# Attention, cosine mixing and gated attention on one core: the order of the steps for all engines, written out

## The chip, the cores and the metric

One core of one Trainium2 chip runs the whole program. The metric is the device time of one execution in microseconds (us), as the median of several runs. Durations and waits are read from one profiled execution of the kernel.

## The reference

The program computes three layers in a row, all in fp32, for 4 batches of 576 tokens with 512 channels:

```
# layer 1: 8 heads of 64; heads 0-3 see the last 32 tokens, heads 4-7 every 32nd token
scores = where(mask[h], q @ k.T / 8, -1e9);  x = softmax(scores) @ v
# layer 2: mixing with a cosine and a sine
theta = x @ w_theta;  zr, zi = x * cos(theta), x * sin(theta)
u = x + w_tok_r @ zr + w_tok_i @ zi
x = u + max(u @ w_ch, 0)
# layer 3: 4 causal attention heads ("experts"), two of which are chosen for each token
w = softmax over the 2 largest of (x @ w_gate)
out = sum over e of w[e] * softmax(causal(x @ wq[e] @ (x @ wk[e]).T / 8)) @ (x @ wv[e]) @ wo[e]
```

## The kernel before, in words

**Tiling.** Tokens lie in five tiles (four of 128 and one of 64), channels in four chunks of 128. Large products are split: each fp32 operand is kept as a high and a low part, and `split_matmuls` (L1271 and on; the matmul itself is L1278) issues three matmuls, hi by hi, hi by lo and lo by hi, in place of one. Transposes and the attention products are plain fp32 matmuls.

**Software pipeline.** Layer 1 of batch r runs together with layer 3 of batch r-1. The program is a PROLOGUE (layers 1 and 2a of batch 0, and the loading and splitting of the weights), three times a BODY (the channel product, q, k, v and layer 3 of one batch, with layers 1 and 2a of the next), and an EPILOGUE (the rest for the last batch). Each is one list of steps. Every engine walks the same list through its own `emit` and does its share of each step, in the order of the list; a step that has nothing for an engine is passed over. So the list fixes the order of the instructions on each of the queues (PE, DVE, ACT, POOL, and SP for the loads), and nothing reorders them. Data goes from engine to engine by semaphores.

**PSUM.** There are three pairs of buffers, `wide` (2 banks each), `turned` and `acc`. `Counts.take` hands them out by turns in the order of the list, and a step on PE waits until the use before of its buffer has been read.

**The steps.** A unit of attention is ("s1", pair) in layer 1, with four units, or ("s3", group, pair) in layer 3, with five: group 0 holds token tiles 0 to 2, group 1 tile 3, group 2 tile 4 with both pairs of heads at once. The steps of a unit:

- prep, tail: PE transposes q and k (L1311, L1322). copied: ACT and DVE copy them out (L878, L1028).
- scores: masks and products on PE (L1335, L1350; in layer 3 L1371, L1376).
- max: DVE, for one of two heads (L1045, L1049). exp: ACT, with the sums (L895, L902).
- norm: DVE makes the reciprocal of the sum. For head 0 it also scales the probabilities itself (L1070, L1080); for head 1 POOL scales them (L814, L823).
- turn: PE transposes the probabilities (L1391, L1404), ACT and DVE copy them out to `pt` (L910, L1093).
- values: PE multiplies them by v (L1421, L1447), DVE copies the result out (L1106, or L1116 and L1118). xu (layer 1): ACT and POOL split it into high and low parts (L921, L833).

The other steps are large products on PE with an eviction of their own: channel, qk, v, theta, out and wtok. Their eviction stands in the list as a step of its own, `("done", ...)`. theta's eviction is three DVE operations (L1125, L1128, L1130), of which the second frees the buffer. A theta product has four chunks, each of three matmuls, and can be cut: ("theta", m, 0, 2) is the first two chunks. trig is ACT (L942, L943), products is a transpose on PE (L1489) and two DVE products (L1140, L1142), split is ACT and POOL (L958, L840), wave and mix are the token products on PE. piece splits a part of the weights (ACT L999, then DVE L1254, or POOL L828 for theta's); SP loads piece n+3 once piece n is split. warm is a number of matmuls whose result nobody reads. rank, gexp and gate choose the experts (DVE, ACT, DVE).

**What sets the order.** `attention_steps` (L89) writes the body by slots: in slot i unit i is ahead (scores, max, exp, norm) and unit i-1 behind (turn, values), and four gaps of the slot are filled from FILL (L262) with the large products. `slot_of_s3` (L137) is the slot of layer 3; `alone_steps` (L178) does the same for the prologue. A gap's product is followed at once by its eviction (`at_once`, L85), except in `slot_of_s3`, which puts the evictions of its first three gaps at the slot's end:

```
    steps = [("turn",) + behind + (0,), ("scores",) + ahead, ("max",) + ahead + (0,), ("max",) + ahead + (1,),
             ("exp",) + ahead + (0,)]
    steps += gap[0] + [("turn",) + behind + (1,), ("norm",) + ahead + (0,), ("exp",) + ahead + (1,)]
    steps += gap[1] + [("values",) + behind] + gap[2] + [("norm",) + ahead + (1,)]
    return steps + done(gap[0] + gap[1] + gap[2]) + at_once(gap[3])
```

The EPILOGUE is already a list that is written out, in both kernels the same.

## Time and profile before

| | us |
|---|---|
| median of 3 runs (lowest to highest) | 575.8 (575.56 to 576.6) |
| the profiled execution | 575.45 |
| its span, first to last instruction | 573.7 |
| PE busy | 545.1 (95%) |
| PE's weight loads (PEld) busy | 467.0 (81%) |
| DVE busy | 348.9 (61%) |
| ACT busy | 259.6 (45%) |
| POOL busy | 130.4 (23%) |

The page cuts the span into 40 slices; the granted clock of TensorE reads 9, which is 90% or more, in all of them, and its mean is 0.999. The profiled execution lies 1.75 us above its span, and 0.35 us below the median of the runs. A PE that shows as busy isn't one at its peak: matmuls overlap, and the ends that the profile shows are modelled. The prologue runs to about 98 us, each body takes 134.8 us, and the epilogue starts at about 502 us.

### The profile page before, as it was taken

The page shows a single profiled execution, that of the slowest core. Times are in us where ns is not written, and L with a number is a line of the kernel's source. Part 1 is how long each engine was busy: PE and PEld are TensorE (multiplying, and loading weights), DVE is VectorE, ACT ScalarE, POOL GpSimd, SP SyncE. Part 2 cuts the span into 40 slices and gives each one's busy share as a digit, 9 for nine tenths or more (in the row PEclk, how much of TensorE's full clock was granted, in tenths as well). Part 3 has the DMA queues.
Part 4 walks back from the last instruction along what each step waited for, and adds up shares of the span by engine and source line. Part 5 has one row for each costly group of instructions (what it writes and reads, how often), then busy time and mean ns, then how long its engine had stood idle before and what let it go on. Part 6 is the DMA issues. An engine that isn't in the chain of part 4 may idle for free.

```text
span 573.7 us, 11679 instructions
## 1 busy us (share of the span) xinstructions
PE 545.1 (95%) x4473; PEld 467.0 (81%) x4473; DVE 348.9 (61%) x843; ACT 259.6 (45%) x775; POOL 130.4 (23%) x131
## 2 busy tenths in 40 slices
PE   6999999999999999999999999999999999999986
PEld 5777889989866799899876689999976679998764
DVE  1677856675888622476678741567677952343683
ACT  2874734555533541355553542255643454121453
POOL 4550710022221250011321152011131126000110
PEclk9999999999999999999999999999999999999999
DMA  9742046221000114211000012331000010000002
GB/s 224 178 115 77 1 112 158 67 49 27 2 0 1 38 47 112 66 43 30 14 1 2 19 65 55 83 83 23 22 1 1 1 75 10 1 2 1 0 1 83
DMA packets 73413, 27.13 MB, mean 47 GB/s; under 512 B 68624, under 2 KB 68624, under 8 KB 73360
## 3 DMA queue, kind: packets, MB, share of 16 engines
q1 hardware_dynamic: 68848, 24.38, 16.7%
q10 hardware_dynamic: 4512, 2.02, 1.3%
q8 instruction: 36, 0.59, 0.4%
q14 instruction: 17, 0.14, 0.1%
HBM read 21.67 MB, written 4.72 MB: 46 GB/s over the span
## 4 chain that ended last, share of the span: by engine, by line
PE 74%; DVE 15%; ACT 5%; issue 3%; POOL 2%; POOLq 0%; DVEq 0%; ACTq 0%
PE acc L1278 33%; PE wide L1278 14%; PE wide L1350 4%; PE turned L1447 4%; PE turned L1391 3%; PE wide L1371 3%; PE turned L1404 2%; DVE xt L1106 2%; PE turned L1421 2%; DVE nmax L1049 2%; PE turned L1489 2%; PE turned L1311 2%; ACT probs L902 2%; PE wide L1335 1%; DVE probs L1080 1%
## 5 line engine op out<-in xcount | busy, mean ns | idle before, releaser
L814 POOL TENSOR_TENSOR probs<-probs,rec 96x768 f32<-96x768 f32 (+1 forms) x16 | 21.7, 1354 | 204.2 <-DVE rec L1064 204.2
L910 ACT ACTIVATE pt<-turned 128x384 f32<-128x384 f32 (+3 forms) x64 | 30.8, 481 | 77.4 <-PE turned L1404 41.4
L895 ACT ACTIVATE probs<-wide,nmax 96x128 f32<-96x128 f32 (+1 forms) x176 | 61.5, 369 | 9.0 <-DVE nmax L1045 8.9
L823 POOL TENSOR_TENSOR probs<-probs,weight 128x128 f32<-128x128 f32 (+4 forms) x36 | 26.9, 767 | 145.9 <-DVE weight L1087 145.9
L902 ACT ACTIVATE probs<-wide,nmax 128x128 f32<-128x128 f32 (+4 forms) x72 | 39.0, 553 | 36.2 <-DVE nmax L1049 25.6
L1278 PE MATMUL wide<-w_tok_hi,z_hi 128*128 128x288 f32 x216 | 47.4, 300 | 0.0
L1278 PE MATMUL wide<-w_tok_hi,z_lo 128*128 128x288 f32 x216 | 46.0, 293 | 0.0
L1278 PE MATMUL wide<-w_tok_lo,z_hi 128*128 128x288 f32 x216 | 45.9, 293 | 0.0
L1049 DVE TENSOR_REDUCE nmax<-wide 128x1 f32<-128x128 f32 (+4 forms) x72 | 33.1, 512 | 13.1 <-PE wide L1376 13.0
L840 POOL TENSOR_TENSOR z_lo<-absf,z_hi 128x512 fp32r<-128x512 f32 x20 | 26.3, 1317 | 63.9 <-ACT z_hi L958 63.9
L1278 PE MATMUL acc<-xu_hi,w_ch_hi 128*128 128x288 f32 x128 | 39.3, 307 | 1.0 <-DVE xu_lo L1176 0.9
L1140 DVE TENSOR_TENSOR absf<-turned,absf 128x512 f32<-128x512 f32 (+1 forms) x20 | 13.7, 686 | 42.6 <-PE turned L1489 42.6
L1278 PE MATMUL acc<-x_hi,w_qk_hi 128*128 128x288 f32 x128 | 39.6, 309 | 0.0
L1045 DVE TENSOR_REDUCE nmax<-wide 96x6 f32<-96x768 f32 (+1 forms) x32 | 27.8, 879 | 17.0 <-PE wide L1350 17.0
L1278 PE MATMUL acc<-xu_hi,w_ch_lo 128*128 128x288 f32 x128 | 37.7, 295 | 0.0
L1278 PE MATMUL acc<-x_lo,w_qk_hi 128*128 128x288 f32 x128 | 37.7, 295 | 0.0
L1278 PE MATMUL acc<-xu_lo,w_ch_hi 128*128 128x288 f32 x128 | 37.7, 294 | 0.0
L1278 PE MATMUL acc<-x_hi,w_qk_lo 128*128 128x288 f32 x128 | 37.7, 294 | 0.0
L895 ACT ACTIVATION_READ_ACCUMULATOR probs<-wide,nmax 96x1 f32 (+1 forms) x176 | 36.8, 209 | 0.0
L1093 DVE COPY pt<-turned 128x288 f32<-128x288 f32 (+4 forms) x72 | 31.9, 452 | 7.2 <-PE turned L1404 4.9
L1278 PE MATMUL acc<-w_theta_hi,xu_hi 128*128 128x512 f32 (+1 forms) x80 | 35.8, 447 | 0.2 <-DVE turns L1128 0.2
L1278 PEld LDWEIGHTS wide<-w_tok_lo,z_hi 128*128 128x128 f32 x216 | 34.4, 188 | 0.0
(190 smaller groups left out, 1458.9 us busy)
## 6 DMA issues: line engine op xcount, KB each, us to landing
raw_q<-in_q SPq DMA_DIRECT2D x32, 128.0 KB, 2.4
out<-o_sb SPq DMA_DIRECT2D x16, 256.0 KB, 2.0
raw_k<-in_k SPq DMA_DIRECT2D x28, 128.0 KB, 2.5
...
stage<-in_moe_w_theta ACTq DMA_DIRECT2D x2, 512.0 KB, 7.5
...
```

Source lines behind the costliest of these rows:

```text
L814: g.tensor_tensor(pr, pr, rec[0:rows, 1, 0:nt].unsqueeze(2).broadcast_to([rows, nt, w]), ALU.mult).then_inc(s["probs_pool"], 1)
L823: ins = g.tensor_tensor(pr, pr, weight[:, j:j + 1].broadcast_to([P, n]), ALU.mult)
L840: g.tensor_tensor(z[1][:, chunk, :], src[:, m, :], z[0][:, chunk, :].bitcast(F32), ALU.subtract).then_inc(s["zl"], 1)
L895: e = a.activation(probs[0:rows, hh, t * P:t * P + w], wide[slot][0:rows, t * P:t * P + w], ACT.Exp, bias=nmax[0:rows, hh, t:t + 1], accum ...
L902: e = a.activation(probs[:, hh, to0:to0 + n], wide[slot][:, at0:at0 + n], ACT.Exp, bias=nmax[:, hh, j:j + 1], accum_out=sums[:, hh, j:j + 1])
L910: ins = a.activation(dst, src, ACT.Copy)
L1045: v_.tensor_reduce(nmax[0:rows, hh, 0:nt], src, AX.X, ALU.max, negate=True)\
L1049: ins = v_.tensor_reduce(nmax[:, hh, j:j + 1], wide[u[0]][:, at0:at0 + TOK[m][1] + TOK[m][2]], AX.X, ALU.max, negate=True)
L1093: ins = v_.tensor_copy(dst, src)
L1278: ins = mm(place, lhs[x], rhs[y](cols), start=first and n == 0, stop=last and n == 2)
L1350: ins = mm(wide[slot][0:n, t * P:t * P + k1 - k0], qt[hd, rows * t:rows * t + n], kt[hd, k0:k1], start=False, stop=True, skip_group_check= ...
L1447: ins = mm(turned[slot][hh * HD:(hh + 1) * HD, to:to + rows], v3[0:n, j, e * HD:(e + 1) * HD], pt[0:n, hh, x:x + rows], start=j == 0, stop ...
```

## The change

The functions that put the lists together are gone, and PROLOGUE and BODY stand there step by step. Both lists hold the same steps as before, with the same arguments (131 and 210 of them); only their order is another, and with it the order of the instructions of every engine, the turns of the PSUM buffers and the point at which each wait stands. SP's order in the body stays as it was. `program`, the EPILOGUE and every instruction are untouched.

```diff
-def attention_steps(units, before, fill):
...
-def slot_of_s3(ahead, behind, gap):
...
-def alone_steps(units, early):
...
-PROLOGUE = [("warm", 3, "acc", 1)] + [PREP[0] + ("acc",)] + PREP[1:] \
...
+PROLOGUE = [
+    ("warm", 3, "acc", 1), ("prep", "s1", 0, 0, "acc"), ("copied", "s1", 0, 0), ("tail", "s1", 0, 0),
+    ("scores", "s1", 0, 0), ("max", "s1", 0, 0, 0), ("max", "s1", 0, 0, 1), ("warm", 1, "acc", 1),
+    ("prep", "s1", 1, 0, "acc"), ("exp", "s1", 0, 0, 0), ("warm", 6, "turned", 0), ("copied", "s1", 1, 0),
+    ("tail", "s1", 1, 0, 2), ("exp", "s1", 0, 0, 1), ("scores", "s1", 1, 0), ("norm", "s1", 0, 0, 0),
+    ("norm", "s1", 0, 0, 1), ("turn", "s1", 0, 0, 0), ("warm", 1, "acc", 1), ("max", "s1", 1, 0, 0), ("piece", 0),
+    ("turn", "s1", 0, 0, 1), ("max", "s1", 1, 0, 1), ("exp", "s1", 1, 0, 0), ("values", "s1", 0, 0),
+    ("prep", "s1", 2, 0, "acc"), ("norm", "s1", 1, 0, 0), ("exp", "s1", 1, 0, 1), ("copied", "s1", 2, 0),
+    ("tail", "s1", 2, 0, 2), ("turn", "s1", 1, 0, 0), ("norm", "s1", 1, 0, 1), ("scores", "s1", 2, 0), ("piece", 1),
+    ("xu", 0), ("max", "s1", 2, 0, 0), ("warm", 1, "acc", 1), ("turn", "s1", 1, 0, 1), ("max", "s1", 2, 0, 1),
+    ("prep", "s1", 3, 0, "acc"), ("exp", "s1", 2, 0, 0), ("weights", 2), ("values", "s1", 1, 0),
+    ("exp", "s1", 2, 0, 1), ("copied", "s1", 3, 0), ("tail", "s1", 3, 0, 2), ("norm", "s1", 2, 0, 0),
+    ("norm", "s1", 2, 0, 1), ("scores", "s1", 3, 0), ("turn", "s1", 2, 0, 0), ("max", "s1", 3, 0, 0),
+    ("warm", 2, "acc", 1), ("xu", 1), ("warm", 2, "acc", 1), ("exp", "s1", 3, 0, 0), ("max", "s1", 3, 0, 1),
+    ("turn", "s1", 2, 0, 1), ("norm", "s1", 3, 0, 0), ("wtok", 0, "acc"), ("values", "s1", 2, 0),
+    ("exp", "s1", 3, 0, 1), ("wtok", 5, "wide"), ("wtok", 1, "wide"), ("norm", "s1", 3, 0, 1),
+    ("done", "wtok", 0, "acc"), ("turn", "s1", 3, 0, 0), ("xu", 2), ("turn", "s1", 3, 0, 1), ("values", "s1", 3, 0),
+    ("theta", 0, 0, 3), ("done", "wtok", 5, "wide"), ("xu", 3), ("theta", 1, 0, 3), ("theta", 0, 3, 4),
+    ("done", "wtok", 1, "wide"), ("wtok", 6, "wide"), ("done", "theta", 0), ("done", "wtok", 6, "wide"),
+    ("theta", 1, 3, 4), ("theta", 2), ("done", "theta", 1), ("theta", 3), ("done", "theta", 2), ("trig", 0),
+    ("products", 0), ("done", "theta", 3), ("theta", 4), ("split", 0), ("trig", 1), ("trig", 2), ("products", 1),
+    ("products", 2), ("done", "theta", 4), ("split", 1), ("trig", 3), ("wave", 0, 0, 0, 2), ("trig", 4),
+    ("wave", 0, 1, 0, 2), ("split", 2), ("products", 3), ("wave", 0, 0, 2, 3), ("wave", 0, 1, 2, 3), ("products", 4),
+    ("split", 3), ("wave", 1, 0), ("split", 4), ("wtok", 2, "turned"), ("done", "wtok", 2, "turned"), ("wave", 1, 1),
+    ("wtok", 7, "turned"), ("done", "wtok", 7, "turned"), ("wave", 2, 0), ("wtok", 3, "turned"), ("piece", 2),
+    ("piece", 3), ("done", "wtok", 3, "turned"), ("wave", 2, 1), ("wtok", 8, "turned"), ("piece", 4), ("wave", 3, 0),
+    ("done", "wtok", 8, "turned"), ("piece", 5), ("wtok", 4, "turned"), ("done", "wtok", 4, "turned"), ("piece", 6),
+    ("wave", 3, 1), ("piece", 7), ("wave", 4), ("mix", 3), ("piece", 8), ("weights", 8),
 ]
-BODY = [("load",)] + attention_steps(S1_UNITS + S3_UNITS, PREP[:1] + at_once(channel(0)) + PREP[1:] + x2(0), FILL) + WAVE[1:]
+BODY = [
+    ("load",), ("prep", "s1", 0, 0), ("channel", 0, 0), ("done", "channel", 0, 0), ("channel", 0, 1),
+    ("done", "channel", 0, 1), ("copied", "s1", 0, 0), ("tail", "s1", 0, 0), ("scores", "s1", 0, 0),
+    ("max", "s1", 0, 0, 0), ("prep", "s1", 1, 0), ("exp", "s1", 0, 0, 0), ("channel", 1, 0), ("channel", 1, 1),
+    ("max", "s1", 0, 0, 1), ("done", "channel", 1, 0), ("x2hi", 0), ("done", "channel", 1, 1), ("exp", "s1", 0, 0, 1),
+    ("x2lo", 0), ("channel", 2, 0), ("x2hi", 1), ("channel", 2, 1), ("norm", "s1", 0, 0, 0),
+    ("done", "channel", 2, 0), ("x2lo", 1), ("copied", "s1", 1, 0), ("done", "channel", 2, 1), ("channel", 3, 0),
+    ("x2hi", 2), ("done", "channel", 3, 0), ("turn", "s1", 0, 0, 0), ("x2lo", 2), ("norm", "s1", 0, 0, 1),
+    ("channel", 3, 1), ("tail", "s1", 1, 0), ("scores", "s1", 1, 0), ("done", "channel", 3, 1), ("x2hi", 3),
+    ("x2lo", 3), ("max", "s1", 1, 0, 0), ("turn", "s1", 0, 0, 1), ("max", "s1", 1, 0, 1), ("v", 0), ("done", "v", 0),
+    ("values", "s1", 0, 0), ("exp", "s1", 1, 0, 0), ("prep", "s1", 2, 0), ("copied", "s1", 2, 0),
+    ("norm", "s1", 1, 0, 0), ("v", 1), ("exp", "s1", 1, 0, 1), ("done", "v", 1), ("tail", "s1", 2, 0), ("v", 2),
+    ("xu", 0), ("turn", "s1", 1, 0, 0), ("scores", "s1", 2, 0), ("norm", "s1", 1, 0, 1), ("done", "v", 2), ("v", 3),
+    ("max", "s1", 2, 0, 0), ("turn", "s1", 1, 0, 1), ("exp", "s1", 2, 0, 0), ("v", 4), ("max", "s1", 2, 0, 1),
+    ("done", "v", 3), ("exp", "s1", 2, 0, 1), ("done", "v", 4), ("values", "s1", 1, 0), ("norm", "s1", 2, 0, 0),
+    ("prep", "s1", 3, 0), ("copied", "s1", 3, 0), ("qk", 0, 0), ("norm", "s1", 2, 0, 1), ("tail", "s1", 3, 0),
+    ("xu", 1), ("scores", "s1", 3, 0), ("turn", "s1", 2, 0, 0), ("qk", 0, 1), ("max", "s1", 3, 0, 0), ("rank", 0, 5),
+    ("done", "qk", 0, 0), ("done", "qk", 0, 1), ("turn", "s1", 2, 0, 1), ("exp", "s1", 3, 0, 0), ("qk", 2, 0),
+    ("max", "s1", 3, 0, 1), ("exp", "s1", 3, 0, 1), ("done", "qk", 2, 0), ("norm", "s1", 3, 0, 0),
+    ("values", "s1", 2, 0), ("qk", 2, 1), ("done", "qk", 2, 1), ("gexp", 0, 5), ("gate", 0, 5),
+    ("norm", "s1", 3, 0, 1), ("xu", 2), ("turn", "s1", 3, 0, 0), ("scores", "s3", 0, 0), ("turn", "s1", 3, 0, 1),
+    ("max", "s3", 0, 0, 0), ("qk", 1, 0), ("max", "s3", 0, 0, 1), ("values", "s1", 3, 0), ("exp", "s3", 0, 0, 0),
+    ("qk", 1, 1), ("done", "qk", 1, 0), ("exp", "s3", 0, 0, 1), ("norm", "s3", 0, 0, 0), ("done", "qk", 1, 1),
+    ("qk", 3, 0), ("done", "qk", 3, 0), ("qk", 3, 1), ("norm", "s3", 0, 0, 1), ("done", "qk", 3, 1), ("xu", 3),
+    ("turn", "s3", 0, 0, 0), ("scores", "s3", 0, 1), ("max", "s3", 0, 1, 0), ("turn", "s3", 0, 0, 1),
+    ("max", "s3", 0, 1, 1), ("exp", "s3", 0, 1, 0), ("theta", 0, 0, 2), ("exp", "s3", 0, 1, 1),
+    ("norm", "s3", 0, 1, 0), ("theta", 0, 2, 3), ("values", "s3", 0, 0), ("norm", "s3", 0, 1, 1), ("theta", 0, 3, 4),
+    ("done", "theta", 0), ("scores", "s3", 1, 0), ("turn", "s3", 0, 1, 0), ("theta", 1, 0, 2), ("theta", 1, 2, 3),
+    ("max", "s3", 1, 0, 0), ("turn", "s3", 0, 1, 1), ("exp", "s3", 1, 0, 0), ("max", "s3", 1, 0, 1),
+    ("norm", "s3", 1, 0, 0), ("exp", "s3", 1, 0, 1), ("norm", "s3", 1, 0, 1), ("theta", 1, 3, 4),
+    ("values", "s3", 0, 1), ("scores", "s3", 1, 1), ("turn", "s3", 1, 0, 0), ("max", "s3", 1, 1, 0),
+    ("theta", 2, 0, 2), ("done", "theta", 1), ("turn", "s3", 1, 0, 1), ("exp", "s3", 1, 1, 0), ("max", "s3", 1, 1, 1),
+    ("exp", "s3", 1, 1, 1), ("theta", 2, 2, 3), ("theta", 2, 3, 4), ("norm", "s3", 1, 1, 0), ("norm", "s3", 1, 1, 1),
+    ("values", "s3", 1, 0), ("scores", "s3", 2, 0), ("done", "theta", 2), ("max", "s3", 2, 0, 0),
+    ("turn", "s3", 1, 1, 0), ("exp", "s3", 2, 0, 0), ("theta", 3, 0, 2), ("turn", "s3", 1, 1, 1), ("theta", 3, 2, 3),
+    ("max", "s3", 2, 0, 1), ("exp", "s3", 2, 0, 1), ("norm", "s3", 2, 0, 0), ("theta", 3, 3, 4), ("done", "theta", 3),
+    ("values", "s3", 1, 1), ("trig", 0), ("out", 0), ("theta", 4, 0, 2), ("done", "out", 0), ("trig", 1),
+    ("norm", "s3", 2, 0, 1), ("turn", "s3", 2, 0, 0), ("theta", 4, 2, 4), ("turn", "s3", 2, 0, 1), ("out", 1),
+    ("done", "theta", 4), ("products", 0), ("done", "out", 1), ("values", "s3", 2, 0), ("out", 2), ("trig", 2),
+    ("done", "out", 2), ("out", 3), ("split", 0), ("trig", 3), ("products", 1), ("done", "out", 3), ("products", 2),
+    ("out", 4), ("done", "out", 4), ("split", 1), ("wave", 0), ("trig", 4), ("split", 2), ("products", 3),
+    ("wave", 1), ("products", 4), ("split", 3), ("split", 4), ("wave", 2), ("wave", 3), ("wave", 4), ("mix", 3),
+]
```

## Rows read from the trace of the kernel before

**Rows 1.** the page, part 1: engine, busy us (share of the span) xinstructions
```profile
PE 545.1 (95%) x4473; PEld 467.0 (81%) x4473; DVE 348.9 (61%) x843; ACT 259.6 (45%) x775; POOL 130.4 (23%) x131
```

**Rows 2.** second body and epilogue: PE, PEld, DVE, ACT, POOL busy, PEclk, DMA, GB/s
```profile
232.80:367.60 134.80, 131.12 (x1098) 112.90 (x1097) 82.81 (x203) 61.03 (x187) 29.14 (x26) 1.00 0.15 38
502.40:573.70 71.30, 62.59 (x516) 52.04 (x514) 39.20 (x126) 23.61 (x61) 6.73 (x9) 1.00 0.05 18
```

**Rows 3.** waits of PE over the whole run: us in total, times, longest us
```profile
PE turned L1447 <- ACT pt L910: 4.3, 9, 0.7
```

**Rows 4.** PE's timeline, second body: start us, us, ..., xcount [idle before <-releaser]
```profile
282.52 0.73 PE L1391 MATMUL turned<-ident,probs 126*126 126x126 f32 x5 [0.15 <-DVE probs L1070]
...
286.01 0.73 PE L1391 MATMUL turned<-ident,probs 126*126 126x126 f32 x5 [0.21 <-POOL probs L814]
...
293.11 0.85 PE L1404 MATMUL turned<-ident,probs 128*128 128x128 f32 x6 [0.27 <-DVE probs L1080]
...
299.53 0.66 PE L1447 MATMUL turned<-pt,v 128*64 128x128 f32 x8 [0.21 <-ACT pt L910]
...
303.94 0.48 PE L1278 MATMUL acc<-w_theta_hi,xu_hi 128*128 128x512 f32 x1
304.26 0.39 PE L1278 MATMUL acc<-w_theta_lo,xu_hi 128*128 128x512 f32 x1
304.49 0.39 PE L1278 MATMUL acc<-w_theta_hi,xu_lo 128*128 128x512 f32 x1
...
307.50 1.53 PE L1447 MATMUL turned<-pt,v 128*64 128x128 f32 x24 [0.54 <-ACT pt L910]
...
314.63 1.09 PE L1447 MATMUL turned<-pt,v 128*64 128x128 f32 x16 [0.41 <-issue]
...
326.91 0.66 PE L1489 MATMUL turned<-ident,xt 128*128 128x128 f32 x4 [0.52 <-ACT pt L910]
```

**Rows 5.** timeline of ACT and DVE around one values step of the second body
```profile
306.29 0.69 ACT L902 ACTIVATE probs<-wide,nmax 128x512 f32<-128x512 f32 x1 [3.47 <-PE turned L1404]
306.96 0.48 ACT L910 ACTIVATE pt<-turned 128x384 f32<-128x384 f32 x1
...
323.19 0.69 DVE L1125 TENSOR_SCALAR absf<-acc 128x512 f32<-128x512 f32 x1
323.91 0.69 DVE L1128 TENSOR_TENSOR turns<-acc,absf 128x512 f32<-128x512 f32 x1
```

**Rows 6.** timeline of DVE and POOL, gate and norm steps of the second body
```profile
282.66 0.17 DVE L1243 SCALAR_TENSOR_TENSOR gate<-rank,gexp 128x20 f32<-128x20 f32 x1
...
283.89 0.16 DVE L1250 COPY gate_last<-gate 64x2 f32<-64x2 f32 x1
...
284.62 1.24 POOL L814 TENSOR_TENSOR probs<-probs,rec 126x630 f32<-126x630 f32 x1 [8.03 <-DVE rec L1064]
```

**Rows 7.** timeline of PE in the prologue
```profile
41.15 0.73 PE L1391 MATMUL turned<-ident,probs 126*126 126x126 f32 x5 [0.41 <-DVE probs L1070]
...
44.60 1.21 PE L1421 MATMUL turned<-pt,raw_v 126*64 126x126 f32 x20 [0.60 <-DVE pt L1093]
...
74.81 0.83 PE L1569 MATMUL turned<-ident,raw_i 128*128 128x128 f32 x5 [1.19 <-DVE w_tok_lo L1258]
```

**Rows 8.** timeline of DVE: the weight pieces, and two norm steps of three tiles
```profile
70.67 3.26 DVE L1254 TENSOR_TENSOR w_vg_lo<-stage,w_vg_hi 128x520 fp32r<-128x520 f32 x2 [1.23 <-ACT w_vg_hi L999]
...
83.63 1.22 DVE L1254 TENSOR_TENSOR w_qk_lo<-stage,w_qk_hi 128x1024 fp32r<-128x1024 f32 x1
...
290.79 2.18 DVE L1080 TENSOR_SCALAR probs<-probs,rec,gate 128x128 f32<-128x128 f32 x3
...
434.41 1.06 DVE L1080 TENSOR_SCALAR probs<-probs,rec,gate 128x128 f32<-128x128 f32 x3
```

**Rows 9.** timeline of POOL beside the longer of the two norm steps
```profile
291.30 1.45 POOL L833 TENSOR_TENSOR xu_lo<-xt,xu_hi 128x576 fp32r<-128x576 f32 x1 [4.06 <-ACT xu_hi L921]
```

**Rows 10.** DMA issues: out<-in, queue, xcount, KB each, median us to landing
```profile
stage<-in_moe_w_ch SPq DMA_DIRECT2D x2, 512.0 KB, 3.8
```

More of the change, by code:

```diff
@@ L76, in chunks @@
     return step[len(result(step)):] or (0, KC)
-def done(steps):
-    return [("done",) + result(x) for x in steps if x[0] in EVICTED and chunks(x)[1] == KC]
-def at_once(steps):
-    return [y for x in steps for y in [x] + done([x])]
-def attention_steps(units, before, fill):
-    steps = list(before)
-    for i in range(len(units) + 1):
-        ahead = units[i] if i < len(units) else None
-        behind = units[i - 1] if i else None
-        nxt = units[i + 1] if i + 1 < len(units) else None
-        gap = list(fill[i]) if i < len(fill) else []
-        gap += [[]] * (4 - len(gap))
-        if behind and behind[0] == "s3":
-            steps += slot_of_s3(ahead, behind, gap) if ahead else last_slot(behind, gap)
-            continue
-        if behind:
-            steps.append(("turn",) + behind + (0,))
-        if ahead:
-            steps += [("scores",) + ahead, ("max",) + ahead + (0,)]
-        if behind:
-            steps.append(("turn",) + behind + (1,))
-        if ahead:
-            steps += [("max",) + ahead + (1,), ("exp",) + ahead + (0,)]
-        steps += at_once(gap[0])
-        if behind:
-            steps.append(("values",) + behind)
-        if nxt and nxt[0] == "s1":
-            steps += [("prep",) + nxt, ("copied",) + nxt]
-        last = bool(behind) and (not ahead or ahead[0] == "s3")
-        if last:
-            steps.append(("xu", behind[1]))
-        if ahead:
-            steps.append(("norm",) + ahead + (0,))
-        steps += at_once(gap[1])
-        if nxt and nxt[0] == "s1":
-            steps.append(("tail",) + nxt)
-        if ahead:
-            steps.append(("exp",) + ahead + (1,))
-        steps += at_once(gap[2])
-        if ahead:
-            steps.append(("norm",) + ahead + (1,))
-        if behind and not last:
-            steps.append(("xu", behind[1]))
-        steps += at_once(gap[3])
-    return steps
@@ L137, in slot_of_s3 @@
-def slot_of_s3(ahead, behind, gap):
-    steps = [("turn",) + behind + (0,), ("scores",) + ahead, ("max",) + ahead + (0,), ("max",) + ahead + (1,),
-             ("exp",) + ahead + (0,)]
-    steps += gap[0] + [("turn",) + behind + (1,), ("norm",) + ahead + (0,), ("exp",) + ahead + (1,)]
-    steps += gap[1] + [("values",) + behind] + gap[2] + [("norm",) + ahead + (1,)]
-    return steps + done(gap[0] + gap[1] + gap[2]) + at_once(gap[3])
-def last_slot(behind, gap):
-    steps = gap[0] + [("turn",) + behind + (0,)] + gap[1] + [("turn",) + behind + (1,)] + gap[2]
-    return steps + [("values",) + behind] + gap[3]
@@ L175 @@
-PREP = [(k,) + S1_UNITS[0] for k in ("prep", "copied", "tail")]
-def alone_steps(units, early):
-    steps = []
-    for i, ahead in enumerate(units):
-        behind = units[i - 1] if i else None
-        nxt = units[i + 1] if i + 1 < len(units) else None
-        if behind:
-            steps.append(("turn",) + behind + (0,))
-        steps += early[i] + [("scores",) + ahead, ("max",) + ahead + (0,)]
-        if behind:
-            steps.append(("turn",) + behind + (1,))
-        steps += [("max",) + ahead + (1,), ("exp",) + ahead + (0,)]
-        steps.append(("warm", 1 if nxt else 2, "acc", 1))
-        if nxt:
-            steps.append(("prep",) + nxt + ("acc",))
-        steps.append(("values",) + behind if behind else ("warm", 6, "turned", 0))
-        steps += [("norm",) + ahead + (0,), ("exp",) + ahead + (1,)]
-        if nxt:
-            steps += [("copied",) + nxt, ("tail",) + nxt + (2,)]
-        else:
-            steps.append(("warm", 2, "acc", 1))
-        steps.append(("norm",) + ahead + (1,))
-        if behind:
-            steps.append(("xu", behind[1]))
-    return steps
```

47 lines of the change are left out of this document (removed).

## The prediction

> **What bounds the kernel now.** I read the page's busy times first. PE is busy for 95% of the span, DVE for 61%, ACT for 45% [rows 1]. So PE's own work is the floor, and an order of steps can only give back the time in which PE stands still. Next come the windows by stretch. A body takes 134.80 us and PE is idle for 3.68 of them; the three bodies are equal within 0.01 us, one stands for all; the epilogue is idle for 8.7, but its list is not changed [rows 2]. PE's waits show who ends the idle time: in most cases an engine that has still to copy a transpose out, as for the nine waits of values for ACT [rows 3]; no load is among them. The timeline of PE shows where: at steps turn and values of layer 3, and at the first products step [rows 4].
>
> Busy time hides a little more. The first row of a theta chunk starts 0.32 before the second, the second 0.23 before the third, while each lasts about 0.39 [rows 4]. So the issue distance is 0.23, the modelled end lies 0.16 behind it, and coming back from a plain fp32 matmul to a split one costs 0.09. A closed wait therefore returns its bracket plus 0.16, less the 0.09 where a switch stays: bracket plus about 0.08.
>
> PEld is busy for 81% only [rows 1]. 512 columns in 0.23 us are 2.2 columns per ns, and the granted clock is 1.00 of the 2.4 GHz level [rows 2, 4], so PE is dense where PEld idles. The Trainium skill (Perfetto Trace Analysis, Identifying the Most-Contended Engine) says that matmul busy is no good measure of headroom and that the busy share of weight loads is; by it a body would have 134.8 - 112.9 = 21.9 us to give. The rows don't bear that out here, and the sum goes by the distances.
>
> **The change, part by part.** No instruction is added or removed. What counts is, for each wait of PE, how much PE work now stands between the step that releases it and the step that needs it.
>
> *Layer 3 of a body, waits that go.* (1) Before each values step PE had one theta chunk (3 x 0.23 = 0.7 us) as cover between turn and values. The copy takes 0.48 and stood behind the exp of the unit ahead (0.69), because the list named that exp first; so values waited 0.54 [rows 4, 5]. Now the second turn is named ahead of that exp, and in four of the five units two chunks (1.4 us) or all three stand before values. The waits of 0.21, 0.54 and 0.41 close. (2) turn s3 0 0 0 waited 0.27 for DVE's norm [rows 4]. Now two more qk halves lie between scores s3 0 0 and it, and values s1 3 comes earlier; it closes. (3) products 0 waited 0.52 for a buffer that ACT had still to read; it now stands behind turn 2 0 1 and out 1, and closes [rows 4]. (4) turn s1 3 0 1 waited 0.21 for POOL [rows 4]; I count it as gone here and as a new wait below. Sum of the six: 0.21 + 0.27 + 0.21 + 0.54 + 0.41 + 0.52 = 2.16, plus 6 x 0.08 = 2.6 us.
>
> *Switches.* Along PE's list a body changes between split products and plain steps 65 times before and 57 times after; four fewer returns at 0.09 are 0.35 us.
>
> *Waits that come.* (5) turn s1 3 0 1 needs POOL's 1.24 us, which needs the reciprocal; that norm now stands behind gate on DVE (282.66 to 284.05, 1.4 us) [rows 6], and the half product (qk 1 0) that used to lie before turn s1 3 0 0 comes only after both turns. From the end of qk 2 1 on PE, DVE needs its eviction and the reciprocal (an estimate, 0.4 each) and 1.4 for gate, and POOL 1.24: 3.4, and 3.9 with four handovers; PE has turn and scores, which took from 282.52 to 286.01 less the wait of 0.21, 3.3 us [rows 4]. I take a wait of 0.6. Bounds: 0, if DVE runs ahead, and 1.4, if all of gate is exposed. (6) theta 4 needs the acc buffer of theta 3, which DVE frees after 1.4 us (0.69 + 0.69, with the gap between) [rows 5]. Before, out 0 and a turn lay between; now theta 3 ends earlier against DVE, and theta 4 follows out 0 directly. DVE has max 2 0 1, norm 2 0 0 and these two operations to do, in sum about 0.4 more than PE has. I take 0.4, bounds 0 and 1.4. The body's total: 2.6 + 0.35 - 1.0 = 1.95; I take 2.0 us. Three bodies: 6.0 us.
>
> *The start of a body, the channel products, v.* The waits at the first scores and at prep after values are set by copies which stand at the same place as before; scores s1 2, s1 3 and prep s1 1 move, but PE was dense there. 0 us, with +0.5 and -0.5 per body as bounds, about one turn or one copy.
>
> *Loads.* SP's order in the body is the same. Its triggers (tail, values) shift by less than 2 us, and PE waited for no load in a body. 0 us. Its cover is the time between a pair's load and its prep, more than 10 us; if that were gone the price would be a landing like the 3.8 us of [rows 10].
>
> *The prologue.* (7) PE waited 1.19 at its second late wtok step, because DVE had split the two vg pieces (3.26 us) before the wtok part that holds the PSUM buffer [rows 7, 8]. Now both pieces come behind two wtok steps. That returns 1.19 + 0.1 = 1.3. The pieces are due later, and with them the loads of pieces 5 to 7; 3.8 us of landing [rows 10] still ends before ACT reaches them, but DVE comes to the eviction of the wave about 0.3 later, just as mix needs the buffer. I take off 0.1: 1.2 us. (8) Among the four units, scores of the next unit go ahead of the turn of the last, which closes waits for norm; at unit 3 PE is about 1.0 ahead. At turn s1 3 0 1 it then waits for POOL, where rows show 0.41 and 0.60 now [rows 7]; I take half of the lead as lost: 0.5 us. Bounds for (8): -1.0 and +2.0. Together 1.7 us.
>
> **Sum.** 6.0 + 1.7 = 7.7 us off the profiled 575.45, and as much off the median, which lies 0.35 above it: 575.8 - 7.7 = 568.1. The epilogue only moves forward.
>
> **Rivals.**
> *A. DVE becomes the one that PE waits for.* In layer 3 every norm, max, copy and theta eviction is DVE's, and PE's walk is shortened by 2 us there. DVE is busy for 82.81 of a body's 134.80 [rows 2], so it has slack on the whole, but in this stretch it has little, and one late eviction holds what is queued behind it. Then (5) and (6) cost double: 2.0 in place of 1.0, a body gives 1.0, the prologue 0.7: 575.8 - 3.7 = 572.1.
> *B. Slower: DVE and POOL meet more often.* A norm of three tiles took 2.18 while POOL ran a subtraction from 291.30 to 292.75, and the same work took 1.06 with POOL idle [rows 8, 9]. The vg pieces took 1.6 each for 520 columns, and 1.22 for 1024 otherwise [rows 8]. So a meeting costs 1.12. If the new order puts three such meetings per body on the path of a turn or of theta's buffer, 3 x 3 x 1.12 = 10.1 against 7.7 gained: 578.2. It decides from the third meeting on (2.0 / 1.12 = 1.8 only cancel a body's gain). Against it: by my reading the norm of the first layer-3 unit comes before POOL's xu 3 and is rid of its meeting. For it: norm of head 0 and head 1 now stand side by side in several units, so POOL runs while DVE goes on.
> The Trainium skill (SBUF — State Buffer, Who interferes with whom) says that a DVE instruction in a two-port mode or with two SBUF inputs and a GpSimd instruction that reads SBUF exclude each other for the whole instruction. The trace agrees with 2.18 against 1.06; at the full 1.45 of the POOL row a meeting would make rival B 581.2.
> *C. More of the gaps close.* No new wait at (5) and (6), prologue +3.5: 3 x 2.95 + 3.5 = 12.4: 563.4.
> *D. Nothing.* The waits move with the steps, and each engine waits at the next one: 575.8.
>
> **How the numbers follow.** The forecast has a chance of 0.5, A 0.2, C 0.14, D 0.04, B 0.12. 0.2% (1.15 us) is about what a measurement of this kernel can tell from no change. Slower by more than that is B: 0.12. Within it: D, and the edges of A: 0.05. Faster: 0.83. The range takes in C and A with their bounds, and leaves out B: 562.0 to 573.5.
>
> **What would show it.** The bodies' length in the windows: 132.8 against 134.8. PE waits at L1447 for ACT, and at L1489, gone or below 0.2 each; a wait of about 0.6 at L1391 for POOL in each body, and a new one of 0.4 at a theta matmul for DVE (turns, L1128). Norm s3 0 0 (L1080, three tiles) at 1.06 in place of 2.18. In the prologue no wait at L1569 for DVE, and the vg pieces under 0.8 each. Wrong: a body at 134 or more, with waits for DVE in layer 3 (A, B), L1080 of three tiles longer than 1.06 (B), or a start of the first body that isn't earlier.

## The result, and the profile after

The kernel after takes 568.08 us (median of 4 runs, 567.49 to 568.11), the kernel before 575.68 in the same comparison; the ratio is 0.9863 [0.9845, 0.988]. The forecast was 568.1. It is right to a tenth of a microsecond, and not for the reasons given: the bodies gave more than the sum said and the prologue gave nothing, and the two errors cancel.

Line numbers of the kernel after are those of before less 112. Part 1 of the page of after, which answers to [rows 1]:

```profile
PE 542.2 (96%) x4473; PEld 468.8 (83%) x4473; DVE 341.6 (60%) x843; ACT 257.9 (46%) x775; POOL 129.4 (23%) x131
```

The windows of the second body and of the epilogue (columns as in [rows 2]):

```profile
230.64:362.64 132.00, 130.02 (x1099) 113.41 (x1098) 80.95 (x203) 60.55 (x187) 29.07 (x26) 1.00 0.16 38
...
494.64:566.00 71.36, 62.66 (x517) 52.11 (x515) 39.24 (x126) 23.59 (x61) 6.73 (x9) 1.00 0.05 18
```

A body takes 132.00 against 134.80: 2.80 less, 8.4 us for three. PE's idle time in a body falls by 1.70 (from 3.68 to 1.98) and its busy time by 1.10, although the instructions are the same: over a third of the gain is in no bracket of a wait. DVE's busy time falls by 1.86 although it does the same work. The epilogue is as it was. But the whole gain is 7.6 in the medians, so the first body must begin later than before. It does. PE's first channel matmul behind its wait for `xu_lo` marks the start of a body, here of the second (its counterpart in the third stands at 364.49):

```profile
232.49 0.40 PE L1166 MATMUL acc<-xu_hi,w_ch_hi 128*128 128x288 f32 x1 [0.29 <-DVE xu_lo L1064]
```

The first of these stands at 100.49 in this profile and at 99.85 in that of before. PE's waits, over the whole run (columns as in [rows 3]):

```profile
PE turned L1335 <- ACT pt L798: 2.0, 3, 0.7
...
PE turned L1279 <- POOL probs L702: 1.6, 4, 0.5
...
PE turned L1309 <- DVE pt L981: 1.5, 2, 0.8
...
PE wide L1223 <- ACT probs L783: 0.7, 1, 0.7
PE turned L1309 <- POOL w_theta_lo L716: 0.7, 1, 0.7
```

The first row answers to [rows 3]: nine waits of 4.3 us in all have become three of 2.0. The six in the bodies are gone; the three that are left lie in the epilogue, whose list is the same. The other four rows are new or larger (the one for DVE's `pt` was one wait of 0.6), and the last three lie in the prologue. PE's timeline has the longest wait of each of these four. The last two rows are the only waits that are left in the second body from the turns of its last layer-1 unit on:

```profile
18.23 0.83 PE L1223 MATMUL wide<-mask_l,ident_b 96*96 96x128 bf16 x6 [0.68 <-ACT probs L783]
...
23.01 1.21 PE L1309 MATMUL turned<-pt,raw_v 96*64 96x96 f32 x24 [0.85 <-DVE pt L981]
...
32.28 1.21 PE L1309 MATMUL turned<-pt,raw_v 96*64 96x96 f32 x24 [0.66 <-POOL w_theta_lo L716]
...
282.28 0.73 PE L1279 MATMUL turned<-ident,probs 126*126 126x126 f32 x5 [0.50 <-POOL probs L702]
...
312.17 1.20 PE L1259 MATMUL wide<-k,q 64*64 64x512 f32 x16 [0.19 <-issue]
```

All brackets of [rows 4] but one are gone; the one at 282.28 (turn s1 3 0 1) has grown from 0.21 to 0.50, and the one of 0.19 at 312.17, ahead of the scores of s3 2 0, is new.

By three stretches the body divides like this. Each length is a difference of two starts on PE: the start of the body, the turn of s3 0 0 0, the first wave, the next start.

| stretch of the second body | before | after |
|---|---|---|
| start to turn s3 0 0 0 | 293.11 - 234.61 = 58.50 | 290.56 - 232.49 = 58.07 |
| to the first wave | 337.61 - 293.11 = 44.50 | 332.32 - 290.56 = 41.76 |
| to the next start | 369.40 - 337.61 = 31.79 | 364.49 - 332.32 = 32.17 |

The last row was in no one's sum: the waves and the mix are the same matmuls in the same order, and they take 0.38 longer.

### The profile page after: what moved, and what is told of

The parts are those of the page before. It is cut to its first block, busy times and chain, and to the rows that moved or that the text cites. A ratio compares the mean times of both kernels' runs of the same rounds, so it can differ in the third digit from the quotient of the medians.

```text
span 566.0 us, 11682 instructions
## 1 busy us (share of the span) xinstructions
PE 542.2 (96%) x4473; PEld 468.8 (83%) x4473; DVE 341.6 (60%) x843; ACT 257.9 (46%) x775; POOL 129.4 (23%) x131
## 4 chain that ended last, share of the span: by engine, by line
PE 83%; DVE 10%; ACT 3%; POOL 2%; issue 2%; POOLq 0%; DVEq 0%
PE acc L1166 40%; PE wide L1166 15%; PE turned L1335 4%; PE wide L1259 4%; PE wide L1238 4%; PE turned L1292 3%; PE turned L1279 3%; PE turned L1309 2%; PE turned L1199 2%; PE turned L1377 2%; PE wide L1223 2%; ACT probs L783 1%; DVE xt L994 1%; DVE nmax L933 1%; DVE pt L981 1%
## 5 line engine op out<-in xcount | busy, mean ns | idle before, releaser
L1166 PEld LDWEIGHTS wide<-w_tok_hi,z_hi 128*128 128x128 f32 x216 | 34.7, 189 | 0.7
L1166 PEld LDWEIGHTS wide<-w_tok_hi,z_lo 128*128 128x128 f32 x216 | 34.7, 189 | 0.0
```

What stands on the lines that cost most here:

```text
L1166: ins = mm(place, lhs[x], rhs[y](cols), start=first and n == 0, stop=last and n == 2)
```

## The experiments

All twelve are orders of the same steps, made from the lists of before and after (the numbers 9 and 10 are not used). In this table "body" is the distance of the starts of the second and the third, "front" the time from PE's first scores to its first theta matmul, and "rest" from there to the first body. Front and rest each repeat to 0.1 us from kernel to kernel where the list is the same (the one exception is the front of E12, 35.64 beside 35.07: in its profile PE waits 0.25 and 0.33 at the two turns of the first unit, where that of before shows no wait), while the first scores themselves start between 10.0 and 11.2 us whatever the list is. So the medians carry a few tenths that no order explains, and front, rest and body tell more.

| kernel | us, median | ratio to before [95%] | body | front | rest |
|---|---|---|---|---|---|
| before | 575.68 | 1 | 134.79 | 35.07 | 54.11 |
| after | 568.08 | 0.9863 [0.9845, 0.988] | 132.00 | 36.59 | 53.08 |
| E1 old prologue | 567.55 | 0.9864 [0.9849, 0.9879] | 131.99 | 35.08 | 54.11 |
| E2 old body | 575.85 | 1.0006 [0.9997, 1.0014] | 134.80 | 36.56 | 53.08 |
| E3 weights late | 567.16 | 0.9858 [0.9845, 0.9872] | 132.03 | 36.21 | 53.00 |
| E4 new layer 3 only | 568.59 | 0.988 [0.9866, 0.9893] | 132.42 | 35.07 | 54.10 |
| E5 norm first | 568.38 | 0.988 [0.9865, 0.9895] | 132.29 | 36.57 | 53.06 |
| E6 one chunk | 571.31 | 0.9929 [0.9917, 0.9942] | 133.19 | 36.63 | 53.01 |
| E7 exp first | 569.11 | 0.989 [0.9877, 0.9904] | 132.40 | 36.57 | 53.01 |
| E8 meeting | 569.83 | 0.99 [0.9887, 0.9914] | 132.68 | 36.57 | 53.07 |
| E11 old tail | 573.39 | 0.9965 [0.9953, 0.9978] | 133.80 | 36.57 | 53.07 |
| E12 joined | 564.2 | 0.98 [0.9787, 0.9814] | 131.30 | 35.64 | 52.70 |
| E13 products late | 562.55 | 0.9778 [0.9764, 0.9791] | 130.80 | 35.07 | 52.68 |
| E14 scalar tail | 564.14 | 0.9804 [0.979, 0.9818] | 131.32 | 35.07 | 52.67 |

### E1 and E2: prologue and bodies apart

```diff
 E1: the kernel after, with
-the PROLOGUE of after
+the PROLOGUE of before
 E2: the kernel after, with
-the BODY of after
+the BODY of before
```

> The prologue of the kernel before, the bodies of the kernel after. Theory (the parts add up: three bodies gain 2.8 us each, the new prologue loses 0.6): 575.7 - 8.3 = 567.4 us, so 0.7 under the kernel after (568.1); the first xu_lo wait of PE ends at 99.85 us as in the kernel before. Rival one, the predicted split (prologue gains 1.7, bodies 2.0 each): 575.7 - 6.0 = 569.7. Rival two, the new prologue hands the bodies something that they need: a body longer than 132.0, and over 568.5 in all.

> The prologue of the kernel after, the bodies of the kernel before. Theory (parts add up): 575.7 + 0.6 = 576.3 us, bodies 134.8 each, the first xu_lo wait ends at 100.5. Rival one, the predicted split, a prologue worth 1.7: 573.9 to 574.0. Rival two, prologue and bodies belong together: over 577. Beside the time: if the slower pace of the wave matmuls (2.40 us for the 18 matmuls of a wave, 2.34 before) comes with the new bodies it is 2.34 here.

Measured: 567.55 and 575.85. The parts add up. The new bodies are as long behind the old prologue (131.99), the old ones behind the new (134.80). The new prologue is worth nothing: E2's ratio is 1.0006, within 0.2% of before. The predicted split would have made them 569.7 and about 574.0. The table says how a prologue with its 1.19 us wait closed can gain nothing: rest is 1.03 shorter, front 1.52 longer, together 0.5 lost.

### E3: the theta weights back where they were

```diff
     ("exp", "s1", 2, 0, 0),
-    ("weights", 2),
     ("values", "s1", 1, 0),
...
+    ("weights", 2),
     ("theta", 0, 0, 3),
```

> The kernel after with one step put back: the copies that round the theta weights, ('weights', 2), stand again right ahead of ('theta', 0, 0, 3) and no longer ahead of ('values', 's1', 1, 0). Theory (the 0.66 us that PE waits for POOL's w_theta_lo ahead of values s1 1 0 is a cost of this move alone): 568.1 - 0.7 = 567.4 us and the wait gone. Rival: the wait is passed on (theta 0 then waits for the same copies, or values s1 1 0 for ACT's copy of its probabilities): 568.1.

Measured: 567.16. The recorded text says that copies are moved; the step holds no copy, only PE's wait for the weight pieces, and POOL's subtraction stands where it stood. In after it ends at 32.22, and PE goes on at 32.28:

```profile
29.86 2.36 POOL L716 TENSOR_TENSOR w_theta_lo<-stage,w_theta_hi 128x1024 fp32r<-128x1024 f32 x1
```

In E3 POOL has the same row at 29.70, PE no longer waits for it, and comes earlier to the scores of s1 3:

```profile
34.39 0.73 PE L1222 MATMUL wide<-mask_s,ident_b 126*126 126x512 bf16 x4 [0.33 <-ACT probs L782]
```

Half is passed on: front shrinks by 0.38, not by 0.66. Theory and rival are each half right. (The median lies 0.9 under that of after; the part beyond 0.4 is in no stretch of PE that the list touches.)

### E4: the first stretch of the body undone

```diff
-the BODY of after up to ("turn", "s3", 0, 0, 0)
+the BODY of before up to ("turn", "s3", 0, 0, 0)
```

> The kernel after with each body's first stretch, up to the turn of s3 0 0 0 (the layers before it, 58.1 us long), in the order of before, and the rest in the new one. Theory (the gain of a body lies by 0.43 us in that stretch, by 2.74 from that turn to the first wave, and 0.38 is lost in the waves): 568.1 + 3 x 0.43 = 569.4 us, bodies 132.4. Rival one, the first stretch costs the 0.21 to 0.50 wait for POOL but gives nothing: 568.1 or just under, 567.5. Rival two, the lost 0.38 of the waves comes from how the first stretch is ordered: then the 18 matmuls of a wave take 2.34 again and the time is 568.3.

The recorded text calls this kernel "after", but the one that ran has the prologue of before as well, so the sum of the theory is 567.4 + 1.3 = 568.7. Measured: 568.59, and a body of 132.42 where 132.4 was expected. The first stretch is worth 0.43. PE's timeline shows its three small waits back, and none of 0.50:

```profile
279.58 0.73 PE L1279 MATMUL turned<-ident,probs 126*126 126x126 f32 x5 [0.16 <-DVE probs L958]
...
283.07 0.73 PE L1279 MATMUL turned<-ident,probs 126*126 126x126 f32 x5 [0.20 <-POOL probs L702]
...
290.18 0.85 PE L1292 MATMUL turned<-ident,probs 128*128 128x128 f32 x6 [0.28 <-DVE probs L968]
```

The waves stay slow, so rival two falls.

### E5: the last norm of layer 1 ahead of the gate

```diff
     ("qk", 2, 1),
+    ("norm", "s1", 3, 0, 1),
     ("done", "qk", 2, 1), ("gexp", 0, 5), ("gate", 0, 5),
-    ("norm", "s1", 3, 0, 1),
```

> The kernel after with one step moved earlier: ('norm', 's1', 3, 0, 1), the sum of a softmax block on DVE and its scaling on POOL, stands ahead of the gate of the same channel block instead of behind it. Theory (PE waits 0.50 us ahead of the turn of s1 3 0 1 because POOL's scaling lies behind the gate's products): the wait is gone and each body 0.50 shorter, 568.1 - 1.5 = 566.6 us, bodies 131.5. Rival: the gate is then late for the rounding of the channel operand and PE waits for that instead: 568.1, or over it.

Measured: 568.38, body 132.29, 0.29 longer. The rival is right. (The norm now stands ahead of the eviction of qk 2 1 as well, not of the gate alone.) The 0.50 wait is gone and two others stand in its place, on PE:

```profile
278.71 0.49 PE L1258 MATMUL wide<-k,q 64*128 64x128 f32 x4 [0.22 <-DVE k L1091]
...
282.31 0.44 PE L1278 MATMUL turned<-ident,probs 126*126 126x126 f32 x2 [0.65 <-DVE pt L980]
```

The first waits for DVE's copy of k, which now stands behind the norm's two small operations. Why the second is so large, DVE shows, beside POOL. In after the gate's seven small operations take 1.4 us while POOL rests, as in [rows 6]:

```profile
278.94 0.17 DVE L1131 SCALAR_TENSOR_TENSOR gate<-rank,gexp 128x20 f32<-128x20 f32 x1
...
280.17 0.16 DVE L1138 COPY gate_last<-gate 64x2 f32<-64x2 f32 x1
```

In E5 POOL works beside them, and two of the seven take seven times as long:

```profile
278.48 1.17 DVE L1130 SCALAR_TENSOR_TENSOR gate<-rank,gexp 128x20 f32<-128x20 f32 x1
279.68 0.18 DVE L1131 TENSOR_REDUCE gden<-gate 128x5 f32<-128x20 f32 x1
279.89 1.10 DVE L1132 TENSOR_SCALAR gden<-gden 128x5 f32<-128x5 f32 x1
```

```profile
278.37 1.24 POOL L701 TENSOR_TENSOR probs<-probs,rec 126x630 f32<-126x630 f32 x1 [7.49 <-DVE rec L951]
279.57 1.40 POOL L720 TENSOR_TENSOR xu_lo<-xt,xu_hi 128x576 fp32r<-128x576 f32 x1
```

The first ends at 279.65 where POOL's operation ends at 279.61, the second at 280.99 where POOL's ends at 280.97; the reduction between them starts beside POOL and isn't held. So moving the norm ahead of the gate lengthens the gate by 1.9 us, and DVE's copy of turned probabilities stands behind it.

### E6 and E7: what closed the waits of values

```diff
 E6: the kernel after, with
+    ("values", "s3", 1, 0),
     ("theta", 2, 3, 4), ("norm", "s3", 1, 1, 0), ("norm", "s3", 1, 1, 1),
-    ("values", "s3", 1, 0),
...
+    ("values", "s3", 1, 1),
     ("theta", 3, 3, 4), ("done", "theta", 3),
-    ("values", "s3", 1, 1),
 E7: the kernel after, with
+    ("exp", "s3", 0, 1, 0),
     ("turn", "s3", 0, 0, 1), ("max", "s3", 0, 1, 1),
-    ("exp", "s3", 0, 1, 0),
...
+    ("exp", "s3", 1, 0, 0),
     ("turn", "s3", 0, 1, 1),
-    ("exp", "s3", 1, 0, 0),
...
+    ("exp", "s3", 1, 1, 0),
     ("turn", "s3", 1, 0, 1),
-    ("exp", "s3", 1, 1, 0),
```

> The kernel after with the values of s3 1 0 and s3 1 1 one piece of theta earlier (one piece, 1.64 us of PE, between softmax and values instead of two), as in the order of before. Theory (what the new order gains there is that second piece, which covers the normalisation and ACT's copy): the waits of before come back, about 0.4 ahead of values s3 1 0 and 0.2 ahead of s3 1 1, 568.1 + 3 x 0.6 = 569.9 us, bodies 132.6. Rival: the copies come early enough by their own order on ACT and the second piece covers nothing: 568.1.

> The kernel after with the first exponentials of s3 0 1, 1 0 and 1 1 named again ahead of the second turn of the block before them, so that ACT does the exponential (0.37 us) before the copy of the turned probabilities. Theory (the copy ahead of the exponential is what took the waits of values): waits of about 0.5 us come back ahead of values in each body, 568.1 + 1.5 = 569.6 us. Rival: the second piece of theta covers the copy in either order: 568.1; and if so, this half of the change buys nothing.

Measured: 571.31 and 569.11, bodies longer by 1.19 and 0.40. In both the waits return at L1335 and L1334. (The text of E6 puts a piece of theta at 1.64; the one moved here is a quarter, 3 matmuls at 0.23 and a switch.) E6, PE's timeline:

```profile
312.21 1.09 PE L1335 MATMUL turned<-pt,v 128*64 128x128 f32 x16 [0.51 <-issue]
318.75 0.99 PE L1335 MATMUL turned<-pt,v 128*64 128x128 f32 x14 [0.27 <-issue]
```

and E7:

```profile
296.98 1.53 PE L1334 MATMUL turned<-pt,v 128*64 128x128 f32 x24 [0.26 <-ACT pt L797]
...
304.95 0.77 PE L1334 MATMUL turned<-pt,v 128*64 128x128 f32 x10 [0.17 <-ACT pt L797]
```

Both halves of the change work, the extra chunk and the copy named ahead of the exponential. The chunk is worth more: its two waits, 0.78 in brackets, cost 1.19, twice the 0.6 expected, and the order on ACT 0.43 in brackets and 0.40 in time. Neither is the price of the waits alone: in both kernels the wait of 0.19 at 312.17 of after is absent, which leaves 0.58 and 0.23 net, and E6 cuts theta 2 once more, with a switch back to it. E7's size was overestimated (1.5 expected, 1.2 in the bodies), since the third wait stays covered.

### E8: the meeting of DVE and POOL brought back

```diff
     ("exp", "s3", 0, 0, 0),
+    ("xu", 3),
     ("qk", 1, 1),
...
     ("done", "qk", 3, 1),
-    ("xu", 3),
     ("turn", "s3", 0, 0, 0),
```

> The kernel after with the channel operand ('xu', 3) named again right behind the first exponential of s3 0 0, so that its addition on POOL meets DVE's normalisation of s3 0 0. By the trace of the kernel before the three tiles then take DVE 2.18 us where they take 1.06 in the kernel after. Theory (PE has some 1.2 us of cover there): DVE's row goes back to 2.18 and the time stays, 568.1 us. Rival (the meeting stands on the path): + 1.1 per body, 571.4 us, with a wait of PE ahead of the turn of s3 0 0 0.

Measured: 569.83, body 132.68: 0.68 a body, between the two. The meeting is there and costs nothing. In after and in E8 the three tiles of DVE's norm read

```profile
287.06 1.06 DVE L968 TENSOR_SCALAR probs<-probs,rec,gate 128x128 f32<-128x128 f32 x3
```

```profile
287.60 2.17 DVE L968 TENSOR_SCALAR probs<-probs,rec,gate 128x128 f32<-128x128 f32 x3
```

and PE has no wait at the turn of s3 0 0 0 in either, since it comes to it 2.0 us after the longer norm has ended (291.75 - 289.77). What costs is the other half of the moved step, ACT's:

```profile
287.35 0.69 ACT L809 ACTIVATE xu_hi<-xt 128x576 fp32r<-128x576 f32 x1 [0.87 <-DVE xt L994]
287.94 0.39 ACT L871 ACTIVATE q<-acc 128x288 f32<-128x288 f32 x1
```

```profile
288.39 0.40 PE L1166 MATMUL acc<-x_hi,w_qk_hi 128*128 128x288 f32 x1 [0.36 <-ACT q L871]
```

`xu_hi` stands ahead of the copy of q, the copy keeps an `acc` buffer, and PE waits for the buffer. The whole 0.68 lies at this spot, although the bracket says 0.36: the first of these matmuls starts 0.64 behind the one before it, where after has 0.13, the next distance is 0.24 for 0.13, and one later 0.21 for 0.13. Rival B's price was right for DVE and its place was wrong.

### E11: the last 41 steps of the body in the old order

```diff
-the BODY of after from its last 41 steps on, which begin with ("theta", 3, 3, 4), ("done", "theta", 3)
+the last 41 steps of the BODY of before, which begin with ("values", "s3", 1, 1), ("theta", 3, 3, 4)
```

> The kernel after with the last 41 steps of each body (from the last piece of theta 3 and the values of s3 1 1 to the end) in the order of before. Theory one, on the products (the new tail takes 0.59 us less of PE from there to the first wave, since nothing stands idle ahead of the second half of theta 4): 3 x 0.59 = 1.8 us more. Theory two, on the pace of the mixing matmuls (130.9 ns each in the kernel before, 133.2 in the kernel after and in every variant of it so far, 0.38 us a body): if the pace hangs on how these 41 steps are ordered it is 130.9 again, and the sum is 568.1 + 1.8 - 1.1 = 568.7 us, bodies 132.2. Rival: the pace hangs on something earlier in the body, stays at 133.2, and the time is 569.9, bodies 132.6.

Measured: 573.39, body 133.80. The pace question is answered: the waves have the fast pace of before again, so what slows them lies in these 41 steps. The time is well over the sum, because the products step doesn't wait 0.52 as in [rows 4] but

```profile
325.38 0.66 PE L1377 MATMUL turned<-ident,xt 128*128 128x128 f32 x4 [1.70 <-ACT pt L798]
```

and on ACT, ahead of the copy that it needs:

```profile
319.67 1.28 ACT L830 ACT_TABLE_LOAD   x1
...
323.77 0.70 ACT L831 ACTIVATE absf<-absf,half_pi 128x512 f32<-128x512 f32 x1
324.38 0.57 ACT L816 ACTIVATE o_sb<-acc 128x512 f32<-128x512 f32 x1
324.86 0.47 ACT L798 ACTIVATE pt<-turned 128x384 f32<-128x384 f32 x1
```

The old list names three sines in a row; with the table load they hold ACT for 4.7 us. Behind the new layer 3 PE comes earlier against ACT, and the wait at the products takes more than half of what was gained: of the 2.8 a body 1.0 is left. The new tail spreads the sines and puts the products behind more work. The sum had priced this step at 0.6.

### E12: the joined kernel

```diff
 the PROLOGUE of before, with
     ("wave", 1, 0), ("split", 4),
-    ("piece", 2), ("piece", 3),
     ("wtok", 2, "turned"), ("done", "wtok", 2, "turned"), ("wave", 1, 1),
...
     ("wave", 2, 0), ("wtok", 3, "turned"),
+    ("piece", 2), ("piece", 3),
 and the BODY of after, with
     ("gexp", 0, 5),
-    ("gate", 0, 5),
     ("norm", "s1", 3, 0, 1), ("xu", 2), ("turn", "s1", 3, 0, 0), ("scores", "s3", 0, 0),
+    ("gate", 0, 5),
```

> The prologue of before up to the second wave and of after from there (pieces 2 and 3 of the weights behind the third transposed token matrix), and the bodies of after with ('gate', 0, 5) moved behind ('scores', 's3', 0, 0), into 2.0 us in which DVE stands idle (281.05 to 283.05 us of the second body), so that the sums of s1 3 0 1 come before it. Theory: against the kernel with the old prologue and the new bodies (567.5) the 1.2 us wait for w_tok_lo goes, and in each body the 0.50 wait for POOL ahead of the turn of s1 3 0 1: 567.5 - 1.2 - 1.5 = 564.8 us, bodies 131.5. Rival one: as when the sums were moved alone, the wait is passed on to DVE's copy of the turned block or to the gate: bodies 132.0 or over, 566.3 or more. Rival two: the pieces lose as much later in the prologue as the wait was worth: 566.0.

The cut shows the main move of the prologue; pieces 4 and 6 and `("wave", 3, 0)` stand as in after too.

Measured: 564.2, rest 52.70 (1.41 less than before), body 131.30 (0.70 less than after). Both parts hold. The gate is stretched by POOL just as in E5, but now into time in which DVE had nothing to do, with the copy of the first turn ahead of it:

```profile
277.49 0.38 DVE L980 COPY pt<-turned 126x252 f32<-126x252 f32 x1
277.79 1.20 DVE L1130 SCALAR_TENSOR_TENSOR gate<-rank,gexp 128x20 f32<-128x20 f32 x1
...
279.24 1.10 DVE L1132 TENSOR_SCALAR gden<-gden 128x5 f32<-128x5 f32 x1
...
281.19 0.42 DVE L980 COPY pt<-turned 126x252 f32<-126x252 f32 x1
```

PE has no wait left between 264.63, in layer 1, and 309.75.

### E13 and E14: the pace of the waves

```diff
 E13: the joined kernel, with
     ("done", "out", 3),
-    ("products", 2),
     ("out", 4), ("done", "out", 4), ("split", 1),
+    ("products", 2),
     ("wave", 0),
 E14: the joined kernel, with
-    ("trig", 3), ("products", 1),
+    ("products", 1),
...
-    ("wave", 0), ("trig", 4), ("split", 2), ("products", 3), ("wave", 1), ("products", 4), ("split", 3), ("split", 4),
+    ("wave", 0), ("split", 2), ("trig", 3), ("products", 3), ("wave", 1), ("split", 3), ("trig", 4), ("products", 4),
+    ("split", 4),
```

> The joined kernel (564.2 us) with ('products', 2) behind the last output block and right ahead of the first wave, so that from the last output block on TensorE's order is that of before. What it tells apart is the pace of the mixing matmuls, 133.2 ns each in every body with the new tail and 130.9 with the old one. Theory one (the pace is set by what TensorE does right ahead of the waves): 130.9 again, 0.38 us less a body, 563.1 us. Rival (it is set by something else): 133.2 and 564.2, or up to 0.4 a body more if the products are then late for their split.

> The joined kernel (564.2 us) with the sines and splits among the waves where they stood in the kernel before (trig 3 and 4 behind splits 2 and 3), so that the order of ACT, DVE and POOL there is that of before and TensorE's is the joined kernel's. Theory one (the pace of the mixing matmuls, 133.2 or 130.9 ns, hangs on when the other engines read and write beside them): 130.9, 563.1 us. Rival: 133.2 and 564.2, or more if a later sine holds up the products.

Measured: 562.55 for E13 and 564.14 for E14, bodies 130.80 and 131.32. Theory one is right for E13, and the rival for E14. The windows of PE from the first matmul behind the last products step to the end of the mix, in before, after, E13 and E14 (length, PE busy, clock, DMA share, GB/s):

```profile
348.07:366.87 18.80, 18.80 (x147) 1.00 0.45 101
```

```profile
342.68:361.96 19.28, 19.28 (x147) 1.00 0.45 101
```

```profile
338.95:357.76 18.81, 18.81 (x147) 1.00 0.44 100
```

```profile
338.83:358.11 19.28, 19.28 (x147) 1.00 0.45 102
```

The same matmuls, the same granted clock, the same DMA share; E11 and E2 have 18.81 too, E12 19.28. The wave ahead of this stretch takes 4.86 to 4.88 us in all of them. So in the bodies the place of one step of four transposes changes the pace of matmuls that begin more than 10 us later, and is worth 0.5 us a body. How it does so, no run here shows: between E12 and E13 the order of PE, ACT, DVE and POOL within the stretch is the same, and the move takes the step behind the last output block and away from products 1 at once.

The pace isn't set once for all waves. On PE's timeline the mean distance between starts (without the larger steps between groups) is, for wave 0, wave 1 and the last stretch: 133.2, 132.9 and 130.0 ns in before, 132.7, 133.0 and 133.3 in after, 129.9, 133.0 and 130.0 in E13. Nor does the order of the steps decide it alone: the 12 `acc` matmuls behind the products 3 of the prologue run at 133.1 ns in before and at 129.7 in E1, with the same prologue. And in the prologue of before, where products 2 stands right ahead of the first wave as in E13, the mix has the slow pace.

## Why the prediction was right, point by point

**The number** was right by cancellation. Predicted: bodies 3 x 2.0 = 6.0, prologue 1.7. Measured: bodies 3 x 2.8 = 8.4, prologue -0.5 by front and rest (-0.6 by the two profiles, -0.3 by E2's ratio).

**(1), values, and (3), products**: right in mechanism, shown by E6, E7 and E11, and too small. The stretch from the turn of s3 0 0 0 to the first wave gave 2.74; the same terms in the sum were 1.68 of brackets with 4 x 0.08, and 0.35 of switches, less 0.4: 1.95. Two things make up most of the 0.8. The wait of (6) isn't there, 0.4. And a wait is worth more than its bracket plus 0.08: 0.68 for 0.36 in E8, where the whole loss lies at one spot, 0.70 for 0.50 in E12, and 0.40 for 0.23 net in E7. E8 has it in parts: 0.51 of distance at the wait, which is the bracket and the 0.16 of the modelled end, then 0.11 and 0.08 behind it. So the rule of bracket plus 0.16 less 0.09 took something off where something comes on top. That this makes up the rest of the 0.8 in the stretch is my reading; no run takes it apart.

**(2), (4), (5), the first stretch**: the sum had 0.21 + 0.27 + 2 x 0.08 - 0.6 = 0.04 for it. Measured 0.43 (E4). The wait of 0.6 came as 0.50, in the place and for the engine named, behind the gate: the best of the small terms. Not in the sum was the wait of 0.15 for DVE ahead of the turn at 282.52, which stood in the rows and closed too. And from `xu` 3, which moved behind the last qk, I expected only DVE's relief. E8 shows that in the new order its ACT half would have cost 0.68 a body had it stayed early.

**(6), theta 4**: wrong. DVE ends its second read of the buffer at 319.50 and PE comes at 319.68 (DVE's and PE's timelines of after):

```profile
318.81 0.69 DVE L1016 TENSOR_TENSOR turns<-acc,absf 128x512 f32<-128x512 f32 x1
```

```profile
319.68 0.39 PE L1166 MATMUL acc<-w_theta_hi,xu_hi 128*64 128x512 f32 x1
```

My count of what DVE has to do in that stretch beyond PE, 0.4, was too high by 0.6. The margin is 0.18, so it was near.

**(7), the wtok wait**: right. The 1.19 is gone and rest is 1.03 shorter, 1.2 predicted; with the old front and the new tail it is 1.41. The two vg pieces together take

```profile
77.83 1.31 DVE L1142 TENSOR_TENSOR w_vg_lo<-stage,w_vg_hi 128x520 fp32r<-128x520 f32 x2
```

against 3.26 in [rows 8].

**(8), the front of the prologue**: this is the step that failed, by its sign: +0.5 predicted, -1.5 measured, outside even the lower bound of -1.0. I had looked at the end of the front (unit 3) and not walked the list from the start. `("weights", 2)` moved from theta 0 to the middle of layer 1; I took it for a step without cost, and E3 shows 0.38 of it. And the scores of s1 1, now ahead of the turn of unit 0, need a `wide` buffer from which ACT still reads: 0.68 at 18.23. The longest is the one at values of unit 0, 0.85 at 23.01 for DVE's copy. In all, PE's waits over 0.15 us between the first scores and theta sum to 4.2 us after and 2.4 before, 1.8 more, against a front that is 1.5 longer. The wait for POOL that I expected at turn s1 3 0 1 isn't there; the waits at the end of the front (0.62, 0.37 and 0.61) are for ACT's and DVE's copies to `pt`. Only the `weights` step was taken apart by a run.

**The waves** weren't in the sum; 0.38 a body, 1.1 in all, is given back there.

**Rivals.** A (DVE becomes the bound): no wait of PE for DVE came to layer 3, though one of 0.85 came to the prologue. B (meetings): the place that I expected to be rid of its meeting is, 1.06 for 2.18, and PE waits for DVE nowhere in layer 3. E5 shows that a meeting on the path is one step away, E8 that one can be hidden whole. C had the bodies right (2.95 each) and the prologue wrong. D falls with the bodies of 132.00.
